# First-layer products of two feature tiles in 15 block products instead of 18, amid the last pair's second layer

## The chip, the cores and the metric

The kernel runs on one core of one Trainium2 chip. The metric is the device time of one launch in microseconds. TensorE (PE in the profile) does the matrix products, VectorE (DVE), ScalarE (ACT) and GpSimd (POOL) the elementwise work, and SyncE (SP) starts the transfers. The five run their own instruction lists and meet only at semaphores. An engine never passes over an instruction that waits: all that stands behind it in the list waits too.

## The reference

The program has three stages: an attention-like recurrence, four experts of two layers each with relu between them, and one wide block of two layers with a gate between them.

```python
def _moe_ref(x, domain_probs, w1, w2) -> np.ndarray:
    N, D = x.shape
    E = w1.shape[0]
    p = domain_probs / (domain_probs.sum(-1, keepdims=True) + 1e-09)
    out = np.zeros((N, D), dtype=np.float32)
    for e in range(E):
        h = np.maximum(x @ w1[e], 0.0)
        out += p[:, e:e + 1] * (h @ w2[e])
    return out.astype(np.float32)

def _moe2_ref(x, w_in, w_out) -> np.ndarray:
    h = x @ w_in
    g = h * (1.0 / (1.0 + np.exp(-1.702 * h)))
    return (g @ w_out).astype(np.float32)
```

There are N = 1536 tokens, D = 384 channels, E = 4 experts of F = 1024 features, and 2048 features in the last block. The change touches neither the recurrence nor expert 0.

## The kernel before

Everything is kept transposed: channels or features on the 128 partitions, tokens along the free axis. The 384 channels are 3 tiles (`KT`), the tokens 3 blocks of 512 (`NB`; expert 0 has the first of them in two spans of 256), and the features of an expert 8 tiles (`FT`). The last block counts as two more stages of 8 tiles. Single precision is made of two float32r parts, `hi` and `lo = x - hi`. A product of two such numbers is three matmuls: hi with hi, hi with lo, and lo with hi (`PASSES`, line 1068).

One step j is one feature tile on one block of tokens. `hidden(j)` (line 1078) is its first layer: 3 channel tiles x 3 passes = 9 matmuls of 512 columns into one of two banks of PSUM (`HID`). `output(j)` (line 1102) is its second layer, 9 matmuls into three banks that add up over all features of the block. PE's list goes hidden(j), output(j-1), hidden(j+1), ... Between the two stand ACT, which writes the relu's high part (line 700), and DVE, which writes its low part from PSUM (line 876). In the last block it is a sigmoid (706), a product (884), a copy (708) and a subtraction (886). After the features of a block DVE multiplies the output by the token's share `p_bc` into one of two `part` buffers (line 866), and POOL adds that to `acc` (631). POOL and ACT also split the next stage's weights into their parts, in pieces of 384 columns (622, 670), and after the last expert the new x (635, 717). The order of all this is written out in the code by loops over j, and for the recurrence by a table that the change leaves alone.

## Time and profile before

| | |
|---|---|
| time, median of 3 runs | 642.78 us (642.29 to 642.92) |
| profiled execution, its span | 640.5 us |
| PE busy | 635.2 us (99%) |
| DVE, ACT, POOL busy | 222.4, 203.4, 170.0 us (35, 32, 27%) |
| granted TensorE clock | 1.000 |

The span is that of one profiled execution, from its first instruction to its last; the time of a launch holds a little more. Busy shares are means over the whole span. An idle engine costs nothing unless another one waits for it. A matmul's listed length runs from its start to its modelled end, and the next one starts before that.

### The profile page before, as it was taken

How to read it: one execution, taken by the hardware profiler on the slowest of the kernel's cores; microseconds unless marked ns; L12 is line 12 of the kernel's file. 1: busy time of each engine (PE TensorE's matmuls, PEld its weight loads, DVE VectorE, ACT ScalarE, POOL GpSimd, SP SyncE). 2: the span in 40 equal slices, each digit the busy share in tenths (PEclk: the TensorE clock that was granted, in tenths of full speed). 3: DMA queues.
4: the chain of work that ended last, by engine and by line, in shares of the span. 5: the costliest groups of instructions: out<-in, count | busy, mean ns of one | idle time of the engine just before them, and what ended most of it. 6: DMA issues, size and time to landing. Idle time of an engine off the chain costs nothing.

```text
span 640.5 us, 9440 instructions
## 1 busy us (share of the span) xinstructions
PE 635.2 (99%) x3880; PEld 529.3 (83%) x3880; DVE 222.4 (35%) x369; ACT 203.4 (32%) x421; POOL 170.0 (27%) x168
## 2 busy tenths in 40 slices
PE   8999999999999999999999999999999999999998
PEld 6999888888888888888888888888888888888886
DVE  8987642212121212121212121213533333333332
ACT  4744432332222212222211223223643333333223
POOL 5664300342242303242402245422750000000000
PEclk9999999999999999999999999999999999999999
DMA  8765521006000501000310000220000010001001
GB/s 331 278 217 189 202 115 51 4 1 247 1 0 1 196 2 49 2 0 1 151 47 1 0 1 0 98 101 1 2 0 1 3 47 1 0 2 50 1 0 50
DMA packets 8722, 39.08 MB, mean 61 GB/s; under 512 B 1504, under 2 KB 1632, under 8 KB 7392
## 3 DMA queue, kind: packets, MB, share of 16 engines
q1 hardware_dynamic: 8672, 38.40, 15.9%
q8 instruction: 33, 0.54, 0.3%
q14 instruction: 17, 0.14, 0.1%
HBM read 36.01 MB, written 2.38 MB: 60 GB/s over the span
## 4 chain that ended last, share of the span: by engine, by line
PE 98%; DVE 1%; DMA 0%; issue 0%; ACT 0%; DVEq 0%
PE bank L1097 46%; PE bank L1123 31%; PE bank L1139 15%; PE bank L1171 2%; PE bank L1215 1%; PE bank L1218 1%; PE bank L1205 1%; PE bank L1190 1%; PE bank L1208 0%; DMA wu_sb<-wu_rows 0%; DVE w_pow L800 0%; DVE q_k_mid L816 0%; PE bank L1223 0%; DVE q_tab_k L807 0%; DVE acc L951 0%
## 5 line engine op out<-in xcount | busy, mean ns | idle before, releaser
L1097 PE MATMUL bank<-x_hi,w_hi 128*128 128x512 f32 (+1 forms) x456 | 172.5, 378 | 0.0
L1097 PE MATMUL bank<-x_lo,w_hi 128*128 128x512 f32 (+1 forms) x456 | 172.4, 378 | 0.0
L1097 PE MATMUL bank<-x_hi,w_lo 128*128 128x512 f32 (+1 forms) x456 | 172.3, 378 | 0.0
L876 DVE SCALAR_TENSOR_TENSOR h_lo<-bank,h_hi 128x512 fp32r<-128x512 f32 (+1 forms) x104 | 67.5, 649 | 257.3 <-ACT h_hi L700 257.3
L700 ACT ACTIVATE h_hi<-bank 128x512 fp32r<-128x512 f32 (+1 forms) x104 | 58.7, 564 | 286.6 <-PE bank L1097 286.6
L622 POOL TENSOR_TENSOR w_lo<-staging,w_hi 128x384 fp32r<-128x384 f32 x80 | 82.2, 1039 | 173.4 <-ACT w_hi L670 173.4
L1123 PE MATMUL bank<-h_hi,w_hi 128*128 128x512 f32 (+1 forms) x312 | 117.7, 377 | 0.1
L1123 PE MATMUL bank<-h_hi,w_lo 128*128 128x512 f32 (+1 forms) x312 | 116.3, 373 | 0.0
L1123 PE MATMUL bank<-h_lo,w_hi 128*128 128x512 f32 (+1 forms) x312 | 116.3, 373 | 0.0
L1097 PEld LDWEIGHTS bank<-x_hi,w_hi 128*128 128x128 f32 x456 | 85.8, 188 | 15.9
L1097 PEld LDWEIGHTS bank<-x_hi,w_lo 128*128 128x128 f32 x456 | 85.8, 188 | 15.8
L1097 PEld LDWEIGHTS bank<-x_lo,w_hi 128*128 128x128 f32 x456 | 85.8, 188 | 15.8
L1123 PEld LDWEIGHTS bank<-h_hi,w_hi 128*128 128x128 f32 x312 | 58.7, 188 | 12.1 <-issue 0.5
L1123 PEld LDWEIGHTS bank<-h_hi,w_lo 128*128 128x128 f32 x312 | 58.7, 188 | 10.3
L1123 PEld LDWEIGHTS bank<-h_lo,w_hi 128*128 128x128 f32 x312 | 58.7, 188 | 10.2
L884 DVE TENSOR_TENSOR acc<-bank,acc 128x512 f32<-128x512 f32 x48 | 33.2, 691 | 90.2 <-ACT acc L706 90.2
L631 POOL TENSOR_TENSOR acc<-acc,part 128x512 f32<-128x512 f32 x27 | 34.2, 1294 | 84.9 <-DVE part L866 84.9
L1139 PE MATMUL bank<-h_lo,w_hi 128*128 128x512 f32 x144 | 56.0, 389 | 0.0
L1139 PE MATMUL bank<-h_hi,w_hi 128*128 128x512 f32 x144 | 56.0, 389 | 0.0
L1139 PE MATMUL bank<-h_hi,w_lo 128*128 128x512 f32 x144 | 56.0, 389 | 0.0
L706 ACT ACTIVATE acc<-bank 128x512 f32<-128x512 f32 x48 | 28.7, 597 | 84.0 <-PE bank L1097 84.0
L670 ACT ACTIVATE w_hi<-staging 128x384 fp32r<-128x384 f32 x96 | 47.2, 516 | 2.9 <-DMA staging<-weights 2.9
(86 smaller groups left out, 433.4 us busy)
## 6 DMA issues: line engine op xcount, KB each, us to landing
staging<-weights SPq DMA_DIRECT2D x10, 1536.0 KB, 8.7
rkv_in<-rkv_n SPq DMA_DIRECT2D x10, 640.0 KB, 5.5
rk_in<-rk_t SPq DMA_DIRECT2D x12, 512.0 KB, 5.2
staging<-weights SPq DMA_DIRECT2D x4, 768.0 KB, 8.9
p_bc<-p_normalised SPq DMA_DIRECT2D x4, 768.0 KB, 4.2
out<-p_bc SPq DMA_DIRECT2D x9, 256.0 KB, 2.1
rkv_in<-rkv_n SPq DMA_DIRECT2D x2, 448.0 KB, 5.7
u_bc<-u_rows SPq DMA_DIRECT2D x1, 192.0 KB, 11.7
```

What stands on the lines that cost most here:

```text
L622: pool.tensor_tensor(part_of(w_lo[s % 2], f, piece), part_of(staging, f, piece), part_of(w_hi[s % 2], f, piece).bitcast(F32), ALU.subtract ...
L631: pool.tensor_tensor(acc[:, k, cols], acc[:, k, cols], part[:, i % 2, :], ALU.add).then_inc(sem["acc"], 1)
L670: act.activation(part_of(w_hi[s % 2], f, piece), part_of(staging, f, piece), ACT.Copy).then_inc(sem["whi"], 1)
L700: act.activation(h_hi[:, j % HRING, 0:size], hid, ACT.Relu).then_inc(sem["hhi"], 1)
L706: act.activation(sig[g % 2], hid, ACT.Sigmoid, scale=1.702).then_inc(sem["sig"], 1)
L876: dve.scalar_tensor_tensor(h_lo[:, slot, 0:size], hid, 0.0, h_hi[:, slot, 0:size].bitcast(F32), ALU.max, ALU.subtract).then_inc(sem["hlo"], 1)
L884: dve.tensor_tensor(gated[g % 2], hid, sig[g % 2], ALU.mult).then_inc(sem["gate"], 1)
L1097: last = pe.matmul(bank[:, HID[j % 2], 0:tokens.stop - tokens.start], w[:, k, :], xs[c][:, k, tokens], start=(n == 0), stop=(n == 3 * KT - 1))
L1123: last = pe.matmul(out_tile(n, k), w[:, k * P:(k + 1) * P], hs[c][:, slot, 0:size],   start=(first and i == 0 and not (n < SMALLS and k == ...
L1139: last = pe.matmul(out_tile(MOE_BLOCKS + b, k), w[:, k * P:(k + 1) * P], hs[c][:, slot, :], start=(first and i == 0), stop=(last_f and i = ...
L1171: last = pe.matmul(bank[:, a_banks(c)[g], p * P:(p + 1) * P], k_mid[rows, c % 2, p, :], r_mid[rows, c % R_RING, p, :], start=True, stop=True)
L1190: last = pe.matmul(kv_of(c)[rows, p * SW + g * D:p * SW + (g + 1) * D], kn_in[:, x, keys], v_in[:, x, p, V_ALL[g]], start=True, stop=True)
```

## The change

The features of experts 1 to 3 and of the last block are taken in pairs of two tiles: 12 pairs for the experts (`MOE_PAIRS`), 8 for the last block, 20 in all. For a pair, the first layer is a product of a 2 x 3 by a 3 x 3 array of blocks (2 feature tiles, 3 channel tiles, 3 blocks of tokens). Done plainly it has 18 block products; the new code does 15, by a scheme of Hopcroft and Kerr, and pair 12 (`PLAIN`) stays plain.

- A block product is three matmuls (`product`, line 1778). Its weight block is one of the tiles or one of 12 sums of tiles that DVE forms for each pair, 128 x 128 each (`weight_sums`, lines 1358 to 1373). Its token block is one of the blocks of x or one of 8 sums, formed once for the experts (`blocks0`) and once for the last block (`blocks1`) by `form` (13 operations on DVE, lines 1316 to 1346), and split by ACT (`sum_high`) and POOL (`sums_low`, line 811).
- The 15 products go into three banks of PSUM (`LONG`, `SHORT`, `ONE`) and are chained there: a product adds to what the bank holds. After each, ACT copies the bank into a tile in SBUF (`t_of`, 6 copies, line 1009) or DVE adds it to one (`join`, 9 additions, lines 1386 and 1388). The next product of the bank waits for that.
- The six finished tiles are then split by ACT and DVE (line 1431, experts), or pass the sigmoid, the gate (line 1425) and a split by ACT and POOL (line 843, last block). All of these read SBUF.
- The second layer of a pair goes in nine groups of six matmuls (`group`, line 1819), three for each block of tokens. For the first block the banks 0 to 2 keep adding up over the pairs of a stage. For the others, banks 3 and 4 in turn are emptied after each group (`leave`, DVE): in the experts through `part`, with `gather` on POOL (line 837), in the last block into `acc2`.
- `pairs()` writes one list for all four engines. In it the products of the next pair stand between the groups of the pair before (`mix`), and the elementwise work some places behind what it reads.

```diff
-SPANS += [(b * NB, NB) for e in range(1, E) for b in range(BLOCKS)]
...
+MOE_PAIRS = (E - 1) * PAIRS_E
+ALL_PAIRS = (STAGES - 1) * PAIRS_E
+PLAIN = MOE_PAIRS
+PRODUCTS = 15
+SUMS = 12
+T_RING, H_RING = 8, 9
...
+ONE, LONG, SHORT = 7, 5, 6
+PRODUCT = (
+    (0, (1, 1), ONE, True, "copy", 1, 1),
...
+    (11, (1, 2), LONG, False, "add", 2, 1),
+)
...
+SUM_ORDER = (13, 8, 14, 3, 9, 1, 10, 4)
...
+        def pairs():
+
+            order = [("product", 0, i) for i in range(PRODUCTS)]
+            begin = {0: 0}
+
+            def mix(q, lead):
+                begin[q + 1] = len(order)
+                left = iter(range(PRODUCTS))
+                for n, takes in enumerate(lead):
+                    if n:
+                        order.append(("group", q, *divmod(n - 1, KT)))
+                    order.extend(("product", q + 1, next(left)) for _ in range(takes))
+
+            for q in range(PLAIN - 1):
+                mix(q, (2, 1, 1, 2, 2, 2, 2, 1, 1, 1))
+            q = PLAIN - 1
+            begin[PLAIN] = len(order)
+            order += [("group", q, n, k) for n in range(2) for k in range(KT)] + [("plain", PLAIN, i) for i in range(2)]
+            order += [("group", q, 2, k) for k in range(KT)] + [("plain", PLAIN, i) for i in range(2, 6)]
+            mix(PLAIN, (0, 0, 0, 0, 0, 2, 1, 2, 2, 8))
+            for q in range(PLAIN + 1, ALL_PAIRS - 1):
+                mix(q, (2, 1, 1, 2, 2, 2, 2, 1, 1, 1))
+            begin[ALL_PAIRS] = len(order)
+            order += [("group", ALL_PAIRS - 1, n, k) for n in range(BLOCKS) for k in range(KT)]
+
+            after = [[] for _ in range(len(order) + 8)]
+            for at, (what, q, *rest) in enumerate(order):
+                if what == "product" and rest[0] in (LAST_OF[o] for o in DONE):
+                    pos = DONE.index(PRODUCT[rest[0]][5])
+                elif what == "plain":
+                    pos = rest[0]
+                else:
+                    if what == "group" and q == PLAIN - 1:
+                        after[at + 2].append(("rest", q, *rest))
+                    continue
+                later = iter(range(at + 1, at + 5))
+                if q >= MOE_PAIRS:
+                    after[next(later)].append(("silu", q, pos))
+                    after[next(later)].append(("gate", q, pos))
+                after[next(later)].append(("high", q, pos))
+                after[next(later)].append(("low", q, pos))
+            for q in range(1, ALL_PAIRS):
+                at = begin[q - 1]
+                if q == PLAIN:
+                    after[at + 4].append(("weight", q, 0))
+                else:
+                    for i, way in enumerate((0, 1, 2)):
+                        after[at + i].append(("sum", q, way))
+                    for i, piece in zip((3, 4, 5, 6, 7), range(len(PIECES))):
+                        after[at + i].append(("weight", q, piece))
+            for q in range(ALL_PAIRS):
+                after[begin[q] + 9].append(("second", q))
+            out = []
+            for at in range(len(after)):
+                out += order[at:at + 1] + after[at]
+            return out
...
-            def split_low(s, f, piece):
-                n = 2 * FT * (s - 1) + 2 * f + piece
-                pool.wait_ge(sem["whi"], 2 * FT + n + 1)
-                pool.tensor_tensor(part_of(w_lo[s % 2], f, piece), part_of(staging, f, piece),
-                                   part_of(w_hi[s % 2], f, piece).bitcast(F32), ALU.subtract).then_inc(sem["wlo"], 1)
-
-            def gather(n):
-
-                e, cols = expert_of(n), slice(SPANS[n][0], sum(SPANS[n]))
-                for k in range(KT):
-                    i = n * KT + k
-                    pool.wait_ge(sem["ev1"], i + 1)
-                    pool.tensor_tensor(acc[:, k, cols], acc[:, k, cols], part[:, i % 2, :], ALU.add).then_inc(sem["acc"], 1)
...
+            def sums_low(turn, blocks):
+
+                for i, op in enumerate(SUM_ORDER):
+                    pool.wait_ge(sem["shi"], len(SUM_ORDER) * turn + i + 1)
+                    pool.tensor_tensor(sum_home(s_lo, x_lo, op), blocks[FORMED[op][0]], sum_home(s_hi, x_hi, op).bitcast(F32),
+                                       ALU.subtract).then_inc(sem["slo"], 1)
...
+            def gather(q, n, k):
+
+                i = LEAVES[q, n, k]
+                pool.wait_ge(sem["evac"], i + 1)
+                cols = slice(n * NB, (n + 1) * NB)
+                pool.tensor_tensor(acc[:, k, cols], acc[:, k, cols], part[:, i % 2, :], ALU.add).then_inc(sem["gath"], 1)
...
+            second_low(0)
+            for what, q, *rest in PAIR_LIST:
+                if what == "group" and (q, *rest) in LEAVES and q < MOE_PAIRS:
+                    gather(q, *rest)
+                elif what == "weight":
+                    weight_low(q, *rest)
+                elif what == "second" and q:
+                    second_low(q)
+                elif what == "low" and q >= MOE_PAIRS:
+                    tile_low(q, *rest)
+                elif what == "plain" and rest[0] == 5:
+                    sums_low(1, blocks1)
...
+            def join(q, i):
+
+                _, _, at, _, _, o, sign = PRODUCT[i]
+                t = t_of[t_number(q, o) % T_RING]
+                before = [x for x in ADDED if x < i and PRODUCT[x][5] == o]
+                dve.wait_ge(sem["prod"], PRODS[q] + i + 1)
+                if before:
+                    dve.wait_ge(sem["added"], JOINED[q] + ADDED.index(before[-1]) + 1)
+                else:
+                    dve.wait_ge(sem["copied"], TAKEN[q] + COPY_OF.index(o) + 1)
+                if sign > 0:
+                    dve.tensor_tensor(t, bank[:, at, :], t, ALU.add).then_inc(sem["added"], 1)
+                else:
+                    dve.scalar_tensor_tensor(t, bank[:, at, :], -1.0, t, ALU.mult, ALU.add).then_inc(sem["added"], 1)
...
+            def leave(q, n, k):
+
+                i = LEAVES[q, n, k]
+                cols = slice(n * NB, (n + 1) * NB)
+                dve.wait_ge(sem["grp"], groups(q, n, k))
+                src = bank[:, KEPT[k] if n == 0 else shared_bank(q, n, k), :]
+                if q < MOE_PAIRS:
+                    if n == 1 and k == 0 or n == 0 and k == 0:
+                        dve.wait_ge(s_prob, 16 * (2 + q // PAIRS_E))
+                    if i >= 2:
+                        dve.wait_ge(sem["gath"], i - 1)
+                    dve.tensor_tensor(part[:, i % 2, :], src, p_bc[:, cols], ALU.mult).then_inc(sem["evac"], 1)
...
+                    dve.tensor_tensor(t, t, part[:, number % 2, :], ALU.mult).then_inc(sem["gate"], 1)
...
+                dve.scalar_tensor_tensor(tile_lo[number % H_RING], t_of[t_number(q, result_of(q, pos)) % T_RING], 0.0,
+                                         tile_hi[number % H_RING].bitcast(F32), ALU.max, ALU.subtract).then_inc(sem["tlo"], 1)
...
+                elif what == "plain" and rest[0] == 5:
+                    form(1, blocks1, 0, FORMINGS)
...
+            def product(q, i):
+
+                weight, rows, at, begins, _, _, _ = PRODUCT[i]
+                piece = next(n for n, (first, last) in enumerate(PIECES) if first <= weight < last)
+                pe.wait_ge(sem["alo"], PARTS_W[q] + piece + 1)
+                if q in (0, PLAIN + 1) and type(rows) is int:
+                    pe.wait_ge(sem["slo"], len(SUM_ORDER) * (q > 0) + SUM_ORDER.index(rows) + 1)
+                if q == PLAIN + 1 and begins and i < 3:
+                    pe.wait_ge(sem["gate"], 6)
+                earlier = [x for x in range(i) if PRODUCT[x][2] == at]
+                if earlier:
+                    x, before = earlier[-1], q
+                elif q and q != PLAIN + 1:
+                    x, before = max(x for x in range(PRODUCTS) if PRODUCT[x][2] == at), q - 1
+                else:
+                    x = None
+                if x in COPIED:
+                    pe.wait_ge(sem["copied"], TAKEN[before] + COPIED.index(x) + 1)
+                elif x in ADDED:
+                    pe.wait_ge(sem["added"], JOINED[before] + ADDED.index(x) + 1)
+                for n, (a, c) in enumerate(PASSES):
+                    last = pe.matmul(bank[:, at, :], a_parts[a][:, q % 2, weight * P:(weight + 1) * P], rows_of(ss[c], xs[c], rows),
+                                     start=(begins and n == 0), stop=(n == 2), skip_group_check=True)
+                last.then_inc(sem["prod"], 1)
...
+            def group(q, n, k):
+
+                begins, ends = (kept_first(q), kept_last(q)) if n == 0 else (True, True)
+                if n == 0:
+                    at = KEPT[k]
+                    if q == 0:
+                        pe.wait_ge(sem["ev1"], KT * len(SPANS))
+                    elif begins:
+                        pe.wait_ge(sem["evac"], LEAVES[q - 1, 0, k] + 1)
+                else:
+                    at = shared_bank(q, n, k)
+                    number = shared_number(q, n, k)
+                    if number >= len(SHARED):
+                        pe.wait_ge(sem["evac"], LEAVES[shared_at(number - len(SHARED))] + 1)
+                pe.wait_ge(sem["vlo"], q + 1)
+                for f in range(2):
+                    number = 6 * q + place_of(q, f, n)
+                    done, value = low_tile(number)
+                    pe.wait_ge(sem[done], value)
+                    for i, (a, c) in enumerate(PASSES):
+                        last = pe.matmul(bank[:, at, :], v_parts[a][q % 2][:, f * DM + k * P:f * DM + (k + 1) * P], tiles[c][number % H_RING],
+                                         start=(begins and f == 0 and i == 0), stop=(ends and f == 1 and i == 2))
+                last.then_inc(sem["grp"], 1)
+
```

How the order changes is shown at three places, by engine. `waits` names the semaphores.

PE. Before, nine matmuls of each layer alternate (`h_` is the hidden tile, `w_` the weights); the rows are the last three of an output and the first three of the next hidden tile.

```order
L1123 MATMUL bank<-h_hi,w_hi11 128x512
L1123 MATMUL bank<-h_lo,w_hi11 128x512
L1123 MATMUL bank<-h_hi,w_lo11 128x512
L1097 MATMUL bank<-x_hi,w_hi00 128x512 [waits s_hlo,s_wlo]
L1097 MATMUL bank<-x_lo,w_hi00 128x512
L1097 MATMUL bank<-x_hi,w_lo00 128x512
```

Now, the end of a pair's products and the start of the next: the last group of the pair before, product 14, and products 0 and 1 of the next pair (the `a_` tensors are the first layer's weights; the group reads hidden tiles and `w_hi00`, the second layer's weights). `s_added` is counted by DVE's joins, `s_tlo` by the tiles' low parts, `s_evac` by the leaves.

```order
L1819 MATMUL bank<-w_lo00,w_hi00 128x512 [waits s_tlo,s_vlo,s_evac]
L1819 MATMUL bank<-w_lo00,w_hi00 128x512 x2
L1819 MATMUL bank<-w_lo00,w_hi00 128x512 [waits s_tlo]
L1819 MATMUL bank<-w_lo00,w_hi00 128x512 x2
L1778 MATMUL bank<-x_hi,a_hi 128x512 [waits s_added,s_alo]
L1778 MATMUL bank<-x_lo,a_hi 128x512
L1778 MATMUL bank<-x_hi,a_lo 128x512
L1778 MATMUL bank<-x_hi,a_hi 128x512 [waits s_added,s_alo]
L1778 MATMUL bank<-x_lo,a_hi 128x512
L1778 MATMUL bank<-x_hi,a_lo 128x512
L1778 MATMUL bank<-s_hi,a_hi 128x512 [waits s_added,s_alo]
```

Each product now waits for the join or copy of the product before it on the same bank (the last row, product 1, for that of product 14, which stands one product back), and the groups wait for the tiles' low parts.

DVE, at the same place: joins (1386, 1388), leaves (1401), low parts of tiles (1431), and then the first of the 12 weight sums (1358 and on). Before, DVE had here only eight low parts in a row and three leaves.

```order
L876 SCALAR_TENSOR_TENSOR h_lo<-bank,h_hi 128x512 [waits s_hhi,s_l1] x8
L866 TENSOR_TENSOR part<-bank,p_bc0 128x512 [waits s_acc,s_prob0,s_l2]
L866 TENSOR_TENSOR part<-bank,p_bc0 128x512 [waits s_acc] x2
L876 SCALAR_TENSOR_TENSOR h_lo<-bank,h_hi 128x512 [waits s_hhi,s_l1] x8
L866 TENSOR_TENSOR part<-bank,p_bc1 128x512 [waits s_acc,s_prob1,s_l2]
```

```order
L1401 TENSOR_TENSOR part<-bank,p_bc 128x512 [waits s_gath,s_grp]
L1388 SCALAR_TENSOR_TENSOR t_rest<-bank,t_rest 128x512 [waits s_copied,s_prod]
L1431 SCALAR_TENSOR_TENSOR w_lo00<-t_most,w_lo00 128x512 [waits s_thi]
L1401 TENSOR_TENSOR part<-bank,p_bc 128x512 [waits s_gath,s_grp]
L1386 TENSOR_TENSOR t_most<-bank,t_most 128x512 [waits s_copied,s_prod]
L1431 SCALAR_TENSOR_TENSOR w_lo00<-t_rest,w_lo00 128x512 [waits s_thi]
L1358 TENSOR_TENSOR staging1<-staging0 128x128 [waits s_alo,s_first1]
L1359 TENSOR_TENSOR staging1<-staging0 128x128
L1361 TENSOR_TENSOR staging1<-staging1,staging0 128x128 [waits s_asum]
```

The join of product 14 (the last 1386) stands behind a leave and a low part, and each operation on a tile in SBUF stands between operations on PSUM.

POOL, at the switch from the experts to the last block. Before, the gathers (631), the new x (635), and the weights of the second half:

```order
L631 TENSOR_TENSOR acc<-acc,part 128x512 [waits s_ev1] x3
L635 TENSOR_TENSOR x_lo<-acc,x_hi 128x512 [waits s_xhi] x3
L631 TENSOR_TENSOR acc<-acc,part 128x512 [waits s_ev1] x3
L635 TENSOR_TENSOR x_lo<-acc,x_hi 128x512 [waits s_xhi] x3
L622 TENSOR_TENSOR w_lo10<-staging0,w_hi10 128x3x128 [waits s_whi]
```

Now: the last gather, the low parts of the plain pair's first two tiles (843), the low parts of the eight sums (811), and the low parts of its other four tiles.

```order
L837 TENSOR_TENSOR acc<-acc,part 128x512 [waits s_evac]
L843 TENSOR_TENSOR w_lo00<-t_most,w_lo00 128x512 [waits s_thi] x2
L811 TENSOR_TENSOR s_lo<-acc,s_hi 128x512 [waits s_shi] x6
L811 TENSOR_TENSOR x_lo<-acc,x_hi 128x512 [waits s_shi] x2
L843 TENSOR_TENSOR w_lo00<-t_most,w_lo00 128x512 [waits s_thi]
L843 TENSOR_TENSOR w_hi01<-t_most,w_hi01 128x512 [waits s_thi] x3
```

The eight low parts of the sums stand between the second and the third tile of the plain pair.

## Rows read from the trace of the kernel before

**Rows 1.** The page, part 1: busy time, share, instructions of each engine.

```profile
PE 635.2 (99%) x3880; PEld 529.3 (83%) x3880; DVE 222.4 (35%) x369; ACT 203.4 (32%) x421; POOL 170.0 (27%) x168
```

**Rows 2.** The page, part 4: shares of the chain that ended last.

```profile
PE 98%; DVE 1%; DMA 0%; issue 0%; ACT 0%; DVEq 0%
```

**Rows 3.** Whom PE waited for: us in total, times, longest.

```profile
PE bank L1053 <- POOL part L513: 1.4, 1, 1.4
PE bank L1171 <- DVE q_r_mid L819: 0.5, 2, 0.3
```

**Rows 4.** The chain in order of time: start, length (us), what.

```profile
502.72 2.04 PE bank L1097 x9
```

**Rows 5.** Groups by form, PE: count, busy us, mean ns, idle before.

```profile
L1097 PE MATMUL bank<-x_lo,w_hi 128*128 128x512 f32 x408 | 158.8, 389 | 0.0
L1139 PE MATMUL bank<-h_lo,w_hi 128*128 128x512 f32 x144 | 56.0, 389 | 0.0
```

**Rows 6.** Timeline of DVE, then POOL, 454 to 463 us: start, length, what.

```profile
455.41 1.43 DVE L886 TENSOR_TENSOR h_lo<-acc,h_hi 128x512 fp32r<-128x512 f32 x1 [0.70 <-ACT h_hi L708]
456.78 0.69 DVE L884 TENSOR_TENSOR acc<-bank,acc 128x512 f32<-128x512 f32 x1
458.17 1.06 DVE L886 TENSOR_TENSOR h_lo<-acc,h_hi 128x512 fp32r<-128x512 f32 x1 [0.70 <-ACT h_hi L708]
...
462.00 1.57 DVE L886 TENSOR_TENSOR h_lo<-acc,h_hi 128x512 fp32r<-128x512 f32 x1 [0.70 <-ACT h_hi L708]
...
454.98 1.31 POOL L635 TENSOR_TENSOR x_lo<-acc,x_hi 128x512 fp32r<-128x512 f32 x1
456.23 2.45 POOL L622 TENSOR_TENSOR w_lo<-staging,w_hi 128x384 fp32r<-128x384 f32 x2
```

**Rows 7.** Lines 884 and 886: ns min/median/max, first and last start.

```profile
L884 DVE TENSOR_TENSOR acc<-bank,acc x48: 681/692/693, 442.3 to 632.0; 128x512 f32<-128x512 f32 x48
...
L886 DVE TENSOR_TENSOR h_lo<-acc,h_hi x48: 691/693/1575, 443.6 to 633.4; 128x512 fp32r<-128x512 f32 x48
```

**Rows 8.** Timeline of POOL, 440 to 475 us: twelve splits without a gap.

```profile
456.23 13.55 POOL L622 TENSOR_TENSOR w_lo<-staging,w_hi 128x384 fp32r<-128x384 f32 x12
```

**Rows 9.** Lines 631 and 622 on POOL: ns min/median/max.

```profile
L631 POOL TENSOR_TENSOR acc<-acc,part x27: 1277/1295/1299, 183.2 to 447.5; 128x512 f32<-128x512 f32 x27
...
L622 POOL TENSOR_TENSOR w_lo<-staging,w_hi x80: 1002/1014/1475, 116.2 to 475.8; 128x384 fp32r<-128x384 f32 x80
```

**Rows 10.** Groups by form, DVE and ACT.

```profile
L876 DVE SCALAR_TENSOR_TENSOR h_lo<-bank,h_hi 128x512 fp32r<-128x512 f32 x88 | 60.8, 691 | 252.9 <-ACT h_hi L700 252.9
...
L708 ACT ACTIVATE h_hi<-acc 128x512 fp32r<-128x512 f32 x48 | 30.4, 633 | 40.1 <-DVE acc L884 40.1
L706 ACT ACTIVATE acc<-bank 128x512 f32<-128x512 f32 x48 | 28.7, 597 | 84.0 <-PE bank L1097 84.0
...
L866 DVE TENSOR_TENSOR part<-bank,p_bc 128x512 f32<-128x512 f32 x27 | 17.8, 687 | 12.5 <-POOL acc L631 7.3 <-PE bank L1123 5.2
...
L901 DVE TENSOR_TENSOR acc<-rkv_in,bank 128x128 f32<-128x128 f32 x1 | 0.3, 273 | 0.0
```

**Rows 11.** Timeline, 215 to 222.5 us: the end of an expert's block.

```profile
214.69 0.39 PE L1123 MATMUL bank<-h_hi,w_lo 128*128 128x512 f32 x1
...
215.12 1.29 DVE L866 TENSOR_TENSOR part<-bank,p_bc 128x512 f32<-128x512 f32 x2 [0.65 <-PE bank L1123]
...
215.89 3.79 POOL L631 TENSOR_TENSOR acc<-acc,part 128x512 f32<-128x512 f32 x3 [0.71 <-DVE part L866]
```

**Rows 12.** Line 932: ns min/median/max with one and with two inputs in SBUF.

```profile
L932 DVE SCALAR_TENSOR_TENSOR part<-part,w_pow,bank x20: 303/306/315, 21.4 to 68.0; 128x96 f32<-128x96 f32 x20
L932 DVE SCALAR_TENSOR_TENSOR part<-part,w_pow,late_kv x12: 310/314/319, 72.9 to 95.5; 128x96 f32<-128x96 f32 x12
```

**Rows 13.** Timeline of PE, 0 to 10 us: the first matmuls.

```profile
1.39 3.60 PE L1053 MATMUL bank<-part 128*128 128x512 bf16 x8 [1.39 <-POOL part L513]
```

**Rows 14.** The page, part 6: count, KB each, us to landing.

```profile
staging<-weights SPq DMA_DIRECT2D x10, 1536.0 KB, 8.7
...
p_bc<-p_normalised SPq DMA_DIRECT2D x4, 768.0 KB, 4.2
```

662 lines of the change are left out of this document (456 added, 206 removed).

## The prediction

> **What bounds the kernel now.** I read the busy shares first [rows 1], then the chain that ended last [rows 2], then who TensorE (PE) waited for [rows 3]. PE is busy for 99% of the span and carries 98% of the chain, and in 640.5 us it waits twice, 1.9 us together. VectorE (DVE) is at 35%, ScalarE (ACT) at 32%, GpSimd (POOL) at 27%. Nothing but PE's own stream sets the end. The reader should see one trap: a 512-column matmul is listed with 389 ns [rows 5], but nine of them take 2.04 us on the chain [rows 4]. They overlap, and each one costs 0.227 us. The median of the runs, 642.78 us, is 2.3 us above the span; I sum against the span and add 2.3.
>
> **What is removed.** P0 to P14 are the products of a pair of feature tiles, g0 to g8 its nine groups of six second-layer matmuls, q the pair's number. A product is 3 matmuls (0.68 us), a group 1.36 us. A pair had 54 first-layer matmuls and has 45; 19 of the 20 pairs change (pair 12 stays plain). 19 x 9 = 171 matmuls x 0.227 = **-38.8 us**. A pair falls from 108 x 0.227 = 24.5 to 22.4 us.
>
> **What is added, and the port.** Per pair DVE now has 9 joins, 6 leaves and 6 tile rests or gates, each 0.69 us [rows 10] with 0.60 from start to start when they stand in a row (two take 1.29 [rows 11]), and 12 sums of 128 columns at 0.27 [rows 10], 0.19 in a row with the same overlap: 21 x 0.60 + 12 x 0.19 = 14.9 us. POOL has six 512-column subtractions or gathers at 1.29 (1.28 in a row), three of 768 columns, and three of 128. From 384 columns at 1.014 and 512 at 1.295 [rows 9] those are 1.84 and 0.46: 7.7 + 5.5 + 1.4 = 14.6 us. ACT has up to 18 tile operations of 0.60 to 0.63 and six weight parts: under 15. All fit in 22.4 us, so no engine is the bound by its sum.
> One thing changes that [rows 6 to 8]. A DVE operation with both inputs in SBUF (L886) has a median of 0.693 us, but 1.43, 1.06 and 1.57 where POOL is running. At 455.41 it lasts until POOL's operation of 454.98 has ended (456.29), plus 0.6. L884, with one input in PSUM, is 0.69 at 456.78 beside the same POOL work, and never above 0.693 in 48 [rows 7]. POOL in turn takes 2.45 us for two operations of 1.01 [rows 6], and 1.13 each over twelve [rows 8]. So such DVE operations and POOL's run one at a time, and the waiting one comes next. The new tile rests, gates, weight sums and block sums are all of this kind, while the rests before (L876) read PSUM. The Trainium skill, page "SBUF — State Buffer", section "Who interferes with whom", says just this: a VectorE instruction with two SBUF inputs contends with a GpSimd one that reads SBUF, and one with at most one SBUF input does not. It speaks against this change; by its opposite the sum is rival A's.
> A second rule would cost more: the "Vector Engine (DVE) Microarchitecture Reference", section "Points that are easy to get wrong", holds that a scalar_tensor_tensor with two non-bf16 SBUF sources runs at half throughput. By it each of the 72 new tile rests of the expert pairs would take about 0.5 us more, and the 11 expert seams, as an estimate, up to 5.5 us together, 673 in the sum. The row disagrees: L932 takes 310 to 319 ns with two SBUF inputs and 303 to 315 with one [rows 12]. I leave it out.
>
> **Seams between pairs.** P1 of the next pair needs the bank of P14, and only P0 (0.68 us) stands between. A consumer starts 0.43 us after the start of the last matmul [rows 11], 0.20 after it would give way to the next; join 14 then takes 0.69. With DVE free P1 starts 0.25 us late. With the port, from the end of P14 as 0: the rest of P11's tile waits for gather g6 until -2.55 and ends -1.95; leave g7 ends -1.27; gather g7 holds the port from -1.23 to 0.05; the rest of P12's tile runs to 0.65, leave g8 to 1.25, join 14 to 1.85. P1 starts 1.2 us late. Bounds 0.25 and 1.2; 11 expert seams, taken at 1.1: **+12.1**. In the last stage POOL's tile rest sits in the gather's place and leaves 0.5: 6 x 0.5 = **+3.0**. After P14 there is room (g0 to g8), so other banks are free in time.
> At the two expert ends (pairs 3 and 7) three more gathers stand before the weight splits. Gathers are then up to 1.5 us late where a leave needs one of two `part` buffers, and the next seam inherits it: 0.5 to 3 each, taken at 1.5: **+3.0**. P7 to P14 of pair 13 stand in a row: **+1.0** (0.5 to 1.5).
>
> **Before pair 0.** In the last block of expert 0, DVE's last four block sums alternate with POOL's first s_lo rests (1.28 us each), so the hidden rest of step 28 ends 2.5 us after PE wants it; 0 to 2.5, taken **+1.5**. Pair 0's products have no groups between. DVE's 12 sums for pair 1 stand before join 3 and wait until pair 0's weights are split, 2.7 us after P0 starts. POOL goes straight on with 1.84 us of second weights, so the sums end at 6.9, join 3 at 7.6, and P6 starts then instead of 3.6. With 0.6 more in the chain: **+4.5** (2.5 if the port were free).
>
> **The switch to the last stage.** Time 0 is the end of P14 of pair 11. PE's own work up to the end of the plain pair is 24.5 us, and to g3 of pair 12 it is 28.6. Plain tiles 0 and 1 need the first block of x: leave (DVE), gather (POOL, 1.28), high part (ACT, 0.63), rest (DVE, two SBUF inputs). DVE has pair 13's 12 weight sums between these, all on the port. By the queues in their order: leave g0 ends 3.8, gather 5.2; leave g1 6.5, gather 7.8; leave g2 9.7, gather 11.0; leave g3 13.3, gather 14.6; the rests of the first block end 11.6, 15.2 and 16.3. Plain 0 starts at 16.4, not 8.2. POOL's first 768-column split waits for ACT, which has the high part of g3 before it (15.2); gathers g4 and g5 end 20.0 and 23.0, g6 (behind the other splits) 28.3, g8 (behind the second-layer split) 34.7. The last rest ends 36.6, and plain 4 and 5 end 40.8: 16.3 late.
> Then DVE's 13 block sums run from 37.9 to 46.0, before the gates of tiles 3 to 5 (48.8). ACT's high part of tile 5 ends 49.4, the first sum's 50.0. POOL's list has the eight s_lo rests before the rests of plain tiles 2 and 3: 8 x 1.28 + 1.6 for the port = 61.9, and two more to 64.5. PE has done g0 to g2 and needs both for g3. So g3 is 64.5 - 28.6 = **+36** late. With a free port the same queues give 32.9 and 54.1: 25.5. I take the port's value, since L886 is stretched in all the rows that meet POOL.
> **Clock.** The kernel's first eight 512-column matmuls take 3.60 us, 0.45 each, though the granted clock reads 1.00 [rows 13]: twice 0.227. PE will now stand idle for 8, 7 and 20 us. If it comes back as at the start, each costs some 1.8: 0 to 5.4, taken **+3.0**.
> Loads are no term: weights land 8.7 us after issue for 1536 KB [rows 14], a pair takes 384 KB twice, over a period ahead. The shares `p_bc` lose their second buffer, but a load lands in 4.2 us and g3 is 10 us off. The tail swaps a 0.60 us copy for a 0.69 us addition.
>
> **Sum.** -38.8 + 12.1 + 3.0 + 3.0 + 1.0 + 1.5 + 4.5 + 36 + 3.0 = +25.3. 640.5 + 25.3 + 2.3 = **668 us**.
>
> **Rivals.**
> A, on the other side: the port doesn't bind, because small or scalar_tensor_tensor operations slip in, or POOL's gaps meet them. Then seams 17 x 0.25 = 4.3, expert ends 1.0, pair 13 0.5, pair 0 2.5, switch 25.5, clock 2: 35.8, so -3.0, 640 us. It decides as soon as all stalls stay under 38.8 us, which needs the switch below some 30. For it: no row shows a scalar_tensor_tensor meeting POOL. Against: [rows 6, 7].
> B: DVE becomes the bound. With 14.9 us of work and 18 port operations a pair, each waiting a full 0.9 us, an expert pair takes 31 us; even 2 us more than I have, over 11 pairs, gives 690. For: DVE serves everything in list order. Against: seam to seam I find POOL idle for some 8 us.
> C: the port is free and the second half of the switch is hidden as well: A's 640 less the 17.1 between 8.4 and 25.5 = 623. Against: PE's list has g3 next, with nothing to pass it.
> That fewer matmuls run than said, or more, I give nothing: the list has 45 for each of the 19 pairs.
>
> **From these to the numbers.** Forecast 0.65, own range 652 to 684; A 0.20; B 0.07; C 0.08. A measurement of this kernel can tell 0.2% (1.3 us) from no change. A splits into 0.15 faster, 0.04 same and 0.01 slower; C is faster; the forecast and B are slower. Faster 0.23, same 0.04, slower 0.73. The range 634 to 686 leaves out C and most of B.
>
> **What would show it.** PE has 3709 matmuls and waits of some 50 to 60 us in all: one of about 20 us before L1819 on POOL's L843, near 490 us, one of about 8 before L1795 on DVE's L1438 and one of about 7 before the fifth plain tile. Seams show as waits of 0.5 to 1.3 us before L1778 on DVE's joins (L1386, L1388), 17 times. L1431 and L1425 have a median near 0.7 and a maximum above 1.8. If L1431 never passes 0.7, the port is wrong and A holds. If PE's wait at L1819 is under 10 us, the list at the switch was misread; if seams are above 2 us, B.

## The result: 5.6% slower, as forecast, by 10 us more than forecast

The changed kernel takes 678.14 us (median of 4 runs, 676.78 to 679.32), the kernel before 642.53 (642.24 to 642.92): ratio 1.0555, 95% interval 1.0539 to 1.0571. Forecast were 668.0 us, 634 to 686, and slower at 0.73. In the profiled execution the span went from 640.5 to 674.9 us, +34.4.

The page of the changed kernel, part 1 (beside [rows 1]) and the shares of the chain (beside [rows 2]):

```profile
span 674.9 us, 10722 instructions
PE 617.0 (91%) x3709; PEld 500.4 (74%) x3709; DVE 502.8 (75%) x864; ACT 294.2 (44%) x578; POOL 388.3 (58%) x318
PE 61%; DVE 18%; POOL 10%; issue 8%; ACT 3%; DMA 1%; DVEq 0%; ACTq 0%; SPq 0%
```

There are 171 matmuls fewer, as planned. But VectorE now has 864 instructions and not 369, and TensorE, which carried 98% of the chain, carries 61%. For whom TensorE waited (us in total, times, longest), beside [rows 3]:

```profile
PE bank L1778 <- DVE t_most L1386: 15.1, 18, 2.8
PE bank L1819 <- POOL w_lo L843: 13.0, 1, 13.0
PE bank L1819 <- DVE part L1401: 6.2, 2, 5.6
PE bank L1795 <- DVE x_lo L1438: 6.1, 1, 6.1
PE bank L1778 <- DVE t_rest L1386: 4.7, 6, 1.1
PE bank L1778 <- DVE t_most L1388: 3.4, 4, 2.7
PE bank L1549 <- DVE h_lo L1148: 1.6, 1, 1.6
```

These seven rows hold 50.1 us; before, it was 1.9 in two. The waits before L1778 are banks that a join has not left yet, 28 of them. The 1.6 stands in the last block of expert 0, ahead of the pairs; the others are the switch to the last stage.

The port, which [rows 6, 7] showed for one form only, is there for the others with two inputs in SBUF. Lines 1431 (rests of the experts' tiles), 1425 (gates) and 1372 (a weight sum), minimum, median and maximum in ns, with L1386 (one input in PSUM) last:

```profile
L1431 DVE SCALAR_TENSOR_TENSOR w_lo<-t_most,w_lo x36: 680/1378/1745, 158.9 to 436.8; 128x512 fp32r<-128x512 f32 x36
L1425 DVE TENSOR_TENSOR t_most<-t_most,part x30: 678/1130/1914, 507.3 to 663.1; 128x512 f32<-128x512 f32 x30
L1372 DVE TENSOR_TENSOR staging<-staging x19: 279/284/1932, 144.6 to 618.1; 128x128 f32<-128x128 f32 x19
L1386 DVE TENSOR_TENSOR t_most<-bank,t_most x70: 674/689/692, 157.5 to 659.7; 128x512 f32<-128x512 f32 x70
```

For L1431 the median is twice the minimum, for L1425 1.7 times: 45 of all 72 rests and 21 of all 42 gates took over 1 us. I had expected medians near 0.7, and a maximum above 1.8, which L1425 has and L1431 (1.745) has not. The weight sums meet GpSimd seldom: 14 of 228 took over 1 us, nearly all the others 0.28.

An expert seam, the end of an expert, and a pair of the last stage in TensorE's timeline (start, length, and in brackets the wait before it), the rows with a wait alone:

```profile
189.65 0.47 PE L1778 MATMUL bank<-s_hi,a_hi 128*128 128x512 f32 x1 [1.08 <-DVE t_most L1386]
213.47 0.47 PE L1778 MATMUL bank<-s_hi,a_hi 128*128 128x512 f32 x1 [1.09 <-DVE t_rest L1386]
...
237.27 0.47 PE L1778 MATMUL bank<-s_hi,a_hi 128*128 128x512 f32 x1 [1.07 <-DVE t_most L1386]
262.74 0.47 PE L1778 MATMUL bank<-s_hi,a_hi 128*128 128x512 f32 x1 [2.78 <-DVE t_most L1386]
...
359.51 0.47 PE L1778 MATMUL bank<-s_hi,a_hi 128*128 128x512 f32 x1 [2.78 <-DVE t_most L1386]
384.87 0.47 PE L1778 MATMUL bank<-s_hi,a_hi 128*128 128x512 f32 x1 [1.08 <-DVE t_most L1386]
...
563.07 0.47 PE L1778 MATMUL bank<-s_hi,a_hi 128*128 128x512 f32 x1 [0.56 <-DVE t_most L1386]
572.39 0.47 PE L1778 MATMUL bank<-s_hi,a_hi 128*128 128x512 f32 x1 [0.23 <-DVE t_most L1388]
575.81 0.47 PE L1778 MATMUL bank<-s_hi,a_hi 128*128 128x512 f32 x1 [0.32 <-DVE t_most L1386]
587.53 0.47 PE L1778 MATMUL bank<-s_hi,a_hi 128*128 128x512 f32 x1 [0.56 <-DVE t_most L1386]
```

A pair is 99 matmuls, 22.44 us at 0.2267. From P1 to P1 it takes 23.82 in an expert, 25.47 over an expert's end (237.27 to 262.74) and 24.46 in the last stage, which has three gaps and not one. A gap costs some 0.25 us more than its length: it counts from a modelled end, 0.39 us after the start of a matmul whose successor would have come at 0.227, and the first matmul after it is followed 0.31 later. I call this 0.25 the restart.

The switch. First TensorE's waits there, then what ran on VectorE, ScalarE and GpSimd in its second half:

```profile
443.06 1.65 PE L1819 MATMUL bank<-w_hi 128*128 128x512 f32 x3 [5.61 <-DVE part L1401]
454.73 1.66 PE L1819 MATMUL bank<-w_lo,w_hi 128*128 128x512 f32 x6 [0.58 <-DVE part L1401]
466.61 0.77 PE L1795 MATMUL bank<-x_hi,a_hi 128*128 128x512 f32 x1 [6.14 <-DVE x_lo L1438]
...
474.85 0.69 DVE L1346 TENSOR_TENSOR acc<-acc 128x512 f32<-128x512 f32 x1
475.46 1.28 DVE L1423 TENSOR_TENSOR t_most<-bank,t_most 128x512 f32<-128x512 f32 x2
478.78 3.21 ACT L973 ACTIVATE s_hi<-acc 128x512 fp32r<-128x512 f32 x6
479.47 7.54 POOL L811 TENSOR_TENSOR s_lo<-acc,s_hi 128x512 fp32r<-128x512 f32 x6 [11.83 <-ACT s_hi L973]
486.96 2.48 POOL L811 TENSOR_TENSOR x_lo<-acc,x_hi 128x512 fp32r<-128x512 f32 x2
489.40 1.26 POOL L843 TENSOR_TENSOR w_lo<-t_most,w_lo 128x512 fp32r<-128x512 f32 x1
490.62 1.27 POOL L843 TENSOR_TENSOR w_hi<-t_most,w_hi 128x512 fp32r<-128x512 f32 x1
490.81 0.77 PE L1819 MATMUL bank<-w_lo,w_hi 128*128 128x512 f32 x1 [12.97 <-POOL w_lo L843]
```

It is the queue that the forecast walked through: block sums, gates, high parts, eight rests, and only then the two rests for the fourth group. The clock behind the waits, in the windows' columns (us, busy PE, PEld, DVE, ACT, POOL, granted clock, DMA share, GB/s):

```profile
443.00:446.00 3.00, 2.94 (x7) 2.39 (x8) 2.28 (x4) 1.24 (x2) 1.65 (x1) 0.50 0.00 0
449.00:464.00 15.00, 10.89 (x47) 8.35 (x45) 5.76 (x9) 7.48 (x13) 10.85 (x10) 1.00 0.08 26
467.00:470.00 3.00, 3.00 (x8) 2.35 (x8) 3.00 (x6) 0.63 (x1) 0.64 (x1) 0.50 0.00 0
491.00:494.00 3.00, 3.00 (x8) 2.27 (x9) 0.25 (x1) 0.00 (x0) 3.00 (x3) 0.50 0.03 5
```

After each of the three long waits the granted clock reads 0.50, that is 1.2 GHz, and the next 13 or 14 matmuls start 0.43 us apart, not 0.227. That costs 2.74, 2.89 and 2.73 us, 8.4 in all.

### The profile page after: what moved, and what is told of

It reads as the page before. It is cut to its first block, busy times and chain, and to the rows that moved or that the text cites. A ratio compares the mean times of both kernels' runs of the same rounds, so it can differ in the third digit from the quotient of the medians.

```text
span 674.9 us, 10722 instructions
## 1 busy us (share of the span) xinstructions
PE 617.0 (91%) x3709; PEld 500.4 (74%) x3709; DVE 502.8 (75%) x864; ACT 294.2 (44%) x578; POOL 388.3 (58%) x318
## 4 chain that ended last, share of the span: by engine, by line
PE 61%; DVE 18%; POOL 10%; issue 8%; ACT 3%; DMA 1%; DVEq 0%; ACTq 0%; SPq 0%
PE bank L1819 22%; PE bank L1778 18%; PE bank L1524 7%; PE bank L1549 7%; POOL acc L837 4%; POOL a_lo L825 3%; DVE t_most L1425 2%; DVE part L1401 2%; PE bank L1580 2%; DVE t_most L1386 2%; DVE w_lo L1431 2%; DVE t_most L1388 2%; DVE staging L1372 1%; POOL s_lo L811 1%; POOL w_hi L830 1%
## 5 line engine op out<-in xcount | busy, mean ns | idle before, releaser
L1819 PE MATMUL bank<-w_lo,w_hi 128*128 128x512 f32 x729 | 189.2, 393 | 13.6 <-POOL w_lo L843 13.0
L1819 PEld LDWEIGHTS bank<-w_lo,w_hi 128*128 128x128 f32 x729 | 137.8, 190 | 44.0 <-issue 13.4
L837 POOL TENSOR_TENSOR acc<-acc,part 128x512 f32<-128x512 f32 x81 | 116.0, 1435 | 62.1 <-DVE part L1401 62.1
L825 POOL TENSOR_TENSOR a_lo<-staging,a_hi 128x128 fp32r<-128x128 f32 (+1 forms) x96 | 100.9, 1081 | 58.9 <-ACT a_hi L990 55.1
L1819 PE MATMUL bank<-w_hi 128*128 128x512 f32 x351 | 95.2, 400 | 5.6 <-DVE part L1401 5.6
L1819 PEld LDWEIGHTS bank<-w_hi 128*128 128x128 f32 x351 | 67.9, 194 | 20.5 <-DVE part L1401 6.0
L1401 DVE TENSOR_TENSOR part<-bank,p_bc 128x512 f32<-128x512 f32 x81 | 55.6, 686 | 35.5 <-PE bank L1819 29.8
L1778 PE MATMUL bank<-s_hi,a_hi 128*128 128x512 f32 x114 | 47.2, 414 | 24.8 <-DVE t_most L1386 14.7
L1009 ACT ACTIVATE t_most<-bank 128x512 f32<-128x512 f32 x84 | 49.7, 593 | 42.5 <-PE bank L1778 41.5
L1778 PE MATMUL bank<-x_hi,a_hi 128*128 128x512 f32 x171 | 67.2, 393 | 0.5 <-DVE t_most L1386 0.4
L1778 PE MATMUL bank<-x_lo,a_hi 128*128 128x512 f32 x171 | 66.6, 390 | 0.0
L1778 PE MATMUL bank<-x_hi,a_lo 128*128 128x512 f32 x171 | 66.6, 389 | 0.0
L1388 DVE SCALAR_TENSOR_TENSOR t_most<-bank,t_most 128x512 f32<-128x512 f32 x56 | 38.5, 688 | 19.5 <-PE bank L1778 18.5
L1778 PEld LDWEIGHTS bank<-s_hi,a_hi 128*128 128x128 f32 x114 | 21.4, 187 | 41.6 <-issue 31.3
L1386 DVE TENSOR_TENSOR t_most<-bank,t_most 128x512 f32<-128x512 f32 x70 | 48.0, 686 | 1.4 <-ACT t_most L1009 1.3
L990 ACT ACTIVATE a_hi<-staging 128x128 fp32r<-128x128 f32 (+1 forms) x95 | 42.5, 514 | 12.7 <-DVE staging L1373 9.7
L1778 PE MATMUL bank<-s_hi,a_lo 128*128 128x512 f32 x114 | 44.8, 393 | 0.0
L1778 PE MATMUL bank<-s_lo,a_hi 128*128 128x512 f32 x114 | 44.7, 392 | 0.0
L1431 DVE SCALAR_TENSOR_TENSOR w_lo<-t_most,w_lo 128x512 fp32r<-128x512 f32 x36 | 41.6, 1155 | 0.7 <-ACT w_lo L1038 0.6
```

Source lines behind the costliest of these rows:

```text
L825: pool.tensor_tensor(new, src, high.bitcast(F32), ALU.subtract).then_inc(sem["alo"], 1)
L837: pool.tensor_tensor(acc[:, k, cols], acc[:, k, cols], part[:, i % 2, :], ALU.add).then_inc(sem["gath"], 1)
L990: act.activation(a_hi[:, q % 2, first * P:last * P], src, ACT.Copy).then_inc(sem["ahi"], 1)
L1009: act.activation(t_of[number % T_RING], bank[:, at, :], ACT.Copy, scale=float(sign)).then_inc(sem["copied"], 1)
L1386: dve.tensor_tensor(t, bank[:, at, :], t, ALU.add).then_inc(sem["added"], 1)
L1388: dve.scalar_tensor_tensor(t, bank[:, at, :], -1.0, t, ALU.mult, ALU.add).then_inc(sem["added"], 1)
```

## The experiments

P0 to P14 are the fifteen block products of a pair. All times stand against the kernel before, run on the same chip (642.33 to 642.64 in each comparison).

**A group between P0 and P1.**

```diff
-                mix(q, (2, 1, 1, 2, 2, 2, 2, 1, 1, 1))
+                mix(q, (1, 2, 1, 2, 2, 2, 2, 1, 1, 1))
```

and the same in the last stage's loop.

> Edit: in each pair's mixed stretch a second-layer group stands between the first two block products (P0, group, P1) instead of P0, P1, group, so that 1.36 us of other matmuls stand ahead of the product whose bank the join of the last pair's P13 frees. Theory T1 (the wait is the distance between a bank's two uses, with a DVE that has room): the 11 expert seams of 1.08 us and the three gaps at expert ends and the pair-0 hand-off's first shrink to under 0.3 each, and the last stage's first gap of 0.56 goes; 11 x 1.3 + 2 x 2.4 + 6 x 0.8 = about -20 us, so 655 to 662 us, ratio to the kernel before about 1.025. Rival R1 (the joins come late because VectorE's accesses of about 1.3 us each behind GpSimd set the pace of the whole pair): the wait only moves to the next product, the seam stays at 0.8 to 1.1 in some other place, time 674 to 678.

663.51 us (662.76 to 664.37), ratio 1.0335 (1.0317 to 1.0352): 14.6 us back. The seams inside an expert are gone, at an expert's end 1.70 us are left, and the last stage has new waits:

```profile
352.18 0.47 PE L1778 MATMUL bank<-s_hi,a_hi 128*128 128x512 f32 x1 [1.70 <-DVE t_most L1386]
...
559.24 0.47 PE L1778 MATMUL bank<-s_hi,a_hi 128*128 128x512 f32 x1 [0.99 <-DVE t_most L1388]
562.64 0.47 PE L1778 MATMUL bank<-s_hi,a_hi 128*128 128x512 f32 x1 [0.31 <-DVE t_most L1386]
```

So the seam is a matter of distance between two uses of a bank, as T1 said. The bank is the one that the join of P14 frees; the expectation names P13 by mistake. T1 asked for too much beside it: the gaps at the expert ends (1.68 and 1.70 left) and at pair 0 (2.75) do not fall under 0.3, and the time is above its range. In the last stage R1 holds in part: a pair still loses 1.3 us plus two restarts, now before P6 and P8.

**The low parts before the block rests.** On GpSimd's list:

```diff
                 elif what == "low" and q >= MOE_PAIRS:
                     tile_low(q, *rest)
-                elif what == "plain" and rest[0] == 5:
-                    sums_low(1, blocks1)
+                    if q == PLAIN and rest[0] == 5:
+                        sums_low(1, blocks1)
```

> Edit: at the switch to the last stage GpSimd takes the low parts of plain pair's six feature tiles (through L843) ahead of the six block rests (L811), not behind them. Theory T1 (the wait of 12.97 us before the fourth second-layer group is the queue of GpSimd: six rests of 1.27 us = 7.5 us and two long splits stand before the low part awaited): the wait before L1819 on L843 falls by 7 to 10 us, the rests of the block sums come later but have groups in front of them; part of it comes back as a wait before L1778 on L811. Time 665 to 671, -7 to -13. Rival R2 (the wait is set by the gates and block sums on VectorE, and the rests are needed next anyway): under 3 us gained, the 12.97 splits into two waits of the same sum.

669.93 us (669.66 to 671.04), ratio 1.0435 (1.0417 to 1.0452): 8.2 us back. The wait of 12.97 is 0.8, and 2.4 and 1.1 have come in its place:

```profile
PE bank L1778 <- issue: 2.4, 1, 2.4
...
PE bank L1819 <- DVE p_bc L1411: 1.1, 1, 1.1
PE bank L1819 <- POOL w_hi L843: 0.8, 1, 0.8
```

**GpSimd only writes.** Left out: the low parts are zeros and the experts are not summed.

```diff
-                pool.tensor_tensor(tile_lo[number % H_RING], t_of[t_number(q, result_of(q, pos)) % T_RING],
-                                   tile_hi[number % H_RING].bitcast(F32), ALU.subtract).then_inc(sem["tlop"], 1)
+                fill(tile_lo[number % H_RING], NB).then_inc(sem["tlop"], 1)
```

where `fill` is three memsets, one after the other, two of the whole tile and one of half of it; and the same in L811, L825, L830 and L837.

> Edit: from the sums of blocks on, GpSimd's subtractions and gathers (two inputs from SBUF) are each replaced by three memsets of the same tile, which only write; the low parts then hold zeros and the experts are not summed, so the output is left out. Everything else, waits and counts included, stands. Theory T1 (VectorE's operations with two SBUF inputs take 1.3 to 1.9 us and not 0.68 because GpSimd's two-input operations hold what both read through): L1431's median falls from 1.35 to 0.68 to 0.75, VectorE's busy time falls by some 60 us or more, the seams before L1778 fall from 1.08 to under 0.4, and the three gaps of each last-stage pair go: 645 to 658 us. Rival R3 (VectorE's time is its own, or GpSimd's writes hold it as much as its reads): L1431 keeps a median over 1.1 and the time stays at 670 to 678.

651.05 us (650.09 to 652.08), ratio 1.0132 (1.0115 to 1.0149): 27.1 us less. The page, part 1, and lines 1439 and 1446, which are L1431 and L1438 of before the edit:

```profile
PE 612.1 (94%) x3709; PEld 500.1 (77%) x3709; DVE 433.6 (67%) x864; ACT 293.4 (45%) x578; POOL 382.0 (59%) x840
...
L1439 DVE SCALAR_TENSOR_TENSOR w_lo<-t_most,w_lo x36: 677/683/693, 156.6 to 421.2; 128x512 fp32r<-128x512 f32 x36
...
L1446 DVE TENSOR_TENSOR x_lo<-acc,x_hi x9: 676/681/693, 423.0 to 448.1; 128x512 fp32r<-128x512 f32 x9
```

GpSimd is as busy as before (382.0 against 388.3), yet VectorE's same 864 instructions take 433.6 us, not 502.8, and none of the pairs' is stretched. It is GpSimd's reading that holds them. The Trainium skill, page "SBUF — State Buffer", section "Who interferes with whom", says that a two-input instruction contends with GpSimd's reads and not with its writes; by that rule the edit frees VectorE, and this trace agrees, maximum 695 ns over the 72 rests of the experts' tiles. Nor is a scalar_tensor_tensor (L1439) slower than a tensor_tensor (L1446) by itself, so the second rule that the forecast weighed was rightly left out.

The wait that grew most is the fourth group's, 15.4 us against 13.0. Counted from the start of the fifth plain tile, TensorE came to it 0.9 us sooner and GpSimd's queue, with three memsets for each subtraction, ended 1.5 later.

**Short gates in the last stage.** Left out: 448 of 512 columns of the gate's product there.

```diff
-                    dve.tensor_tensor(t, t, part[:, number % 2, :], ALU.mult)
+                    dve.tensor_tensor(t[:, 0:64], t[:, 0:64], part[:, number % 2, 0:64], ALU.mult)
```

> Edit: in the last stage (not in the plain pair) the gate's product takes 64 of its 512 columns; the rest of the gating is left out. VectorE so has 42 operations shorter by about 1 us each there, with order, waits and counts as they were. Theory T1 (the three gaps of 0.56, 0.22 and 0.32 us in each last-stage pair come from VectorE being 82% busy there, so joins come late): VectorE's share in 530 to 675 falls to under 70%, the second and third gap go and the first falls under 0.3; a pair takes 22.5 to 22.9 instead of 24.46, time 664 to 669. Rival R4 (the gaps come from bank distance alone, or from the chain join, silu, gate, high, low behind ScalarE): a pair keeps over 24 us, time within 3 us of 678.

672.12 us (672.0 to 672.72), ratio 1.0467 (1.045 to 1.0485): 6.0 us less, not 9 to 14. From the fourth group to the end it takes 177.0 us against 184.1 (670.1 - 493.1 and 674.9 - 490.8); 2.3 us were lost before it, 1.4 of them to the clock at 263.62 (last section). The median is above the range of T1 too. VectorE, in the windows 515 to 640 us, short gates first:

```profile
515.00:640.00 125.00, 122.91 (x535) 99.36 (x534) 97.22 (x173) 70.68 (x130) 78.54 (x64) 1.00 0.08 23
```

```profile
515.00:640.00 125.00, 119.57 (x510) 93.87 (x509) 108.18 (x167) 67.44 (x125) 81.94 (x63) 1.00 0.08 23
```

78% instead of 87%, where I had expected under 70; from pair 15 on the gaps before P6 and P8 are gone, the first falls from 0.56 to 0.20, and a pair takes 22.9 us:

```profile
586.50 0.47 PE L1778 MATMUL bank<-s_hi,a_hi 128*128 128x512 f32 x1 [0.20 <-DVE t_most L1386]
609.41 0.47 PE L1778 MATMUL bank<-s_hi,a_hi 128*128 128x512 f32 x1 [0.20 <-DVE t_most L1386]
```

So those gaps are VectorE's lateness; R4 falls.

**The first two edits together.**

> Edit: the first two edits together (a group between P0 and P1; at the switch GpSimd takes the plain pair's low parts before the block rests). Theory T1 (two separate causes at separate places): the gains add, 678.1 - 14.6 - 8.2 = 655.3, so 654 to 657 us. Rival: they overlap at the switch, since in the first of them the wait before L1819 on L843 rose to 14.5 us and that hides there what comes earlier; then under 3 us below the first edit alone, 660 to 663.

655.89 us (655.04 to 656.89), ratio 1.0207 (1.019 to 1.0224). They add, to 0.6 us.

**Pair 13's weight sums eight places later** (with the two):

```diff
+                    late = 8 if q == PLAIN + 1 else 0
                     for i, way in enumerate((0, 1, 2)):
-                        after[at + i].append(("sum", q, way))
+                        after[at + late + i].append(("sum", q, way))
                     for i, piece in zip((3, 4, 5, 6, 7), range(len(PIECES))):
-                        after[at + i].append(("weight", q, piece))
+                        after[at + late + i].append(("weight", q, piece))
```

> Edit: the former two, and pair 13's twelve weight sums and their splits stand eight places later in the list, behind the hand-over of the gathered blocks. Theory T1 (in the first half of the switch VectorE's evictions L1401 stand behind weight sums of 1.35 us each and GpSimd's gathers L837 behind the splits L825): the waits of 5.6 (L1819 on L1401) and 6.1 us (L1795 on L1438) fall by 2 to 4 us in all, and the slow clock that follows them by 1; part comes back behind the fifth plain tile; 650 to 654 us against 655 for the two edits. Rival R5 (the chain eviction, gather, high part, rest of about 3.3 us a block sets it, whatever else is queued): no change within 1 us of the two edits, or a loss of 2 to 5 us as the sums collide with the forming of the blocks in the second half.

656.08 us (653.44 to 658.3), ratio 1.0198 (1.0168 to 1.0227): nothing gained, as R5 had it. The wait of 5.6 fell to 1.9, as T1 said, and one of 8.5 stands before the fifth plain tile instead of 6.1.

**The fourth gate amid the block sums** (with the first two edits):

```diff
                 elif what == "gate":
                     tile_gate(q, *rest)
+                    if q == PLAIN and rest[0] == 3:
+                        form(1, blocks1, 6, FORMINGS)
...
-                    form(1, blocks1, 0, FORMINGS)
+                    form(1, blocks1, 0, 6)
```

> Edit: the first two, and VectorE takes the gate of the plain pair's fourth tile after six of the thirteen block sums, not after all. Theory T1 (with the low parts first, the fourth group still waits for the gates, which stand behind 4 to 9 us of block sums): the plain pair's fourth tile is ready 4 us sooner, some of it is given back since the last sums come as much later; 652 to 655 us. Rival R6 (the sums' rests are what ends last, before the seventh and eighth group): time as for the two edits or 1 us worse.

658.04 us (657.8 to 658.33), ratio 1.0243 (1.0226 to 1.026): 2 us worse than the two. T1 is refuted; R6 is nearer, though it had at most 1 us. The fourth group's wait fell from 1.05 to 0.56, and the sixth group waits 4.2 us, where it waited 1.1, for the bank that a copy of VectorE (L1411) leaves.

**All of these, and pair 12's second-layer split behind the last gather.**

> Edit: all the edits before it, and the second-layer weights' split of the plain pair two places later, behind the last gather. Theory T1: the gains of the two halves of the switch add to those of the first two edits, 647 to 651 us, still above the kernel before's 642.4, because the last stage's pairs and the forming of sums over again remain. Rival: a piece moved late in the first half collides with the second, 652 to 657 us. Both put it above the kernel before.

654.61 us (653.57 to 657.68), ratio 1.0195 (1.0162 to 1.0227): no gain that can be told from the first two edits. Its timeline shows why the first half gave it back:

```profile
443.70 0.63 ACT L1046 ACTIVATE x_hi<-acc 128x512 fp32r<-128x512 f32 x1 [1.73 <-POOL acc L838]
...
445.01 1.36 DVE L1372 TENSOR_TENSOR staging<-staging 128x128 f32<-128x128 f32 x1
...
448.11 1.88 DVE L1374 TENSOR_TENSOR staging<-staging 128x128 f32<-128x128 f32 x1
...
449.91 1.79 DVE L1439 TENSOR_TENSOR x_lo<-acc,x_hi 128x512 fp32r<-128x512 f32 x2
```

The high part of the block is there at 444.3; its rest starts at 449.9, behind weight sums of 128 columns that take 1.4 to 1.9 us each beside GpSimd, where alone they take 0.28.

**The sums behind that rest, and the block sums whole again.** `late` is 11 for the sums and 9 for their splits.

> Edit: lead and low parts as in the two edits together; the plain pair's second-layer split two places later; pair 13's weight sums on VectorE eleven places later (behind the last gathered block's rest), their splits nine later; the block sums in one piece again. Theory T1 (when the sums stood eight places later they lay right in front of the last two x_lo rests: one x_hi was there at 444.3 and its rest began at 449.9, behind five sums of 1.35 to 1.89 us, and PE waited 9 us before the fifth plain tile): that wait falls from 9 to 3 to 5 us, the first stays near 1.9 instead of 5.6; against the two edits alone (655.9) 648 to 652 us. Rival R7 (whatever is taken out of the first half of the switch must be done in the second, where VectorE has to form the block sums and gates): the fifth plain tile comes sooner but the fourth group waits as much longer, 654 to 657 us.

657.88 us (655.25 to 659.55), ratio 1.0246 (1.0224 to 1.0267). The median is 2.0 above the first two edits, and the ranges overlap. R7 holds in kind: the fifth plain tile waits 5.3 instead of 9.05, but 3.9 and 2.0 come before the fourth and a later group and 2.7 further on. Work moved out of one half of the switch is paid in the other.

**Another order in the last stage** (on top of that):

```diff
             for q in range(PLAIN + 1, ALL_PAIRS - 1):
-                mix(q, (1, 2, 1, 2, 2, 2, 2, 1, 1, 1))
+                mix(q, (1, 2, 1, 1, 1, 2, 2, 2, 2, 1))
```

> Edit: as the one before it, and in the last stage's pairs the block products stand as 1,2,1,1,1,2,2,2,2,1 among the nine groups instead of 1,2,1,2,2,2,2,1,1,1: two groups, not one, and P4 and P5 between them, separate P3 from P6, whose bank P3's join frees. Theory T1 (the gaps of 1.0 and 0.31 us before P6 and P8 come from where VectorE's queue stands at that point, not from its total load of some 80%): both gaps go, 6 x 1.3 = 8 us less than the kernel before it. Rival R8 (VectorE's load there sets the pace, whatever the order): the wait turns up before P11 or P12 or at the next seam, within 2 us of the kernel before it.

652.47 us (651.3 to 655.5), ratio 1.0165 (1.0135 to 1.0195), 5.4 below the one before it, not 8. The waits on L1388 went from 5.7 us to 2.7, those on L1386 from 6.1 to 4.6; waits of up to 0.4 us on ScalarE's copies (L1009) came in. A pair takes 23.60 us, not 24.46. So the queue's place in the list decided 0.9 of the 2.0 us that a pair lost, with VectorE about as loaded as before (82% against 85% from 505 to 640 us); R8 falls. Between P3 and P6 the new order has three groups and two products, not the two groups of the expectation; the order before it had two and two.

**The three edits that gained.** P0, group, P1; the low parts first; the last stage's order.

> Edit: the first two edits (a group between P0 and P1; the low parts before the block rests) and the last stage's order 1,2,1,1,1,2,2,2,2,1, with the weight sums of pair 13 where the changed kernel has them. Theory T1 (the gains of separate places add, and moving the weight sums gained nothing): 655.9 - 5.4 = 650.5 us, 649 to 652, still 1.0% over the kernel before. Rival: it ties with the kernel before within 0.3% (641 to 645), which would need 6 us more than the places just named held.

653.77 us (653.72 to 656.62), ratio 1.019 (1.0165 to 1.0214): above the 649 to 652 expected, and above the kernel before. By the medians the last stage's order gave only 2.1 us here. No correct variant beats the kernel before; the interval of the best, 1.0135 to 1.0195, is clear of 1.

**The same, with GpSimd only writing** (left out as above).

> Edit: the same, with GpSimd's subtractions and gathers replaced by memsets that only write, as once before (low parts are zeros and the experts are not summed, so the output is left out). Theory T1 (what is still lost against the kernel before is mostly VectorE slowed by GpSimd's reads): 651.0 for the writes alone, less 9 to 12 for the low parts first (its wait of 15.4 us was that one), less 1 to 2 for the two orders: 637 to 642 us, at or under the kernel before. Rival R9 (the chain of operations at the switch costs as much whatever they take): 645 to 650 us, at most 5 us under the same kernel with subtractions.

632.43 us (632.3 to 633.3), ratio 0.9847 (0.9831 to 0.9864). 21.3 us less than the same kernel with subtractions, and less than the kernel before; R9 falls, and T1 (637 to 642) asked for too little. From pair 15 to pair 18 TensorE then loses nothing. With a GpSimd that only writes this order would win by 1.5%; with its reads none of the nine correct orders did.

## Why the prediction was right, and where its size was off

By stage, in us over the pure matmul time (2.04 / 9 = 0.2267 us for each). The last column takes differences of TensorE's starts in the trace, less what the kernel before has up to the same place.

| step of the forecast | forecast | measured |
|---|---|---|
| 171 matmuls fewer | -38.8 | -38.8 |
| last block of expert 0, and pair 0 up to P1 of pair 1 (165.9) | 1.5 + 4.5 | 7.4 |
| expert pairs, P1 to P1: 165.87 to 408.64, ten of 22.44 | 12.1 + 3.0 | 18.4 |
| switch, up to the fourth group of pair 12 | 36 + 3 | 31.9 |
| last stage from there | 1.0 + 3.0 | 15.5 |
| sum | +25.3 | +34.4 |

The matmuls saved are shown by their number. The waits of the first measured term (1.58, 2.74, 0.22, 0.47, 0.20, 0.27) sum to 5.5; restarts and shorter stops are the rest.

*The port.* Right, and stronger than I took it. The forecast had an operation with two SBUF inputs meeting GpSimd now and then, with medians near 0.7; 45 of 72 tile rests and 21 of 42 gates took over 1 us. The kernel with memsets shows it: the same instructions, 69 us less of VectorE, 27 us less in all. Rival A needed a port that doesn't bind; with such a port this kernel gives 651.05, where A said 640, so even A's condition would not have made it faster with its lists as they were: its four waits at the switch still sum to 25.3 us.

*Expert pairs.* The mechanism (P1 waits for the bank that the join of P14 frees) is shown by the group put in between. The wait was right, 1.08 for 1.1; the restart of 0.25 us a gap was not in the sum. At an expert's end the extra over a seam was 1.65 for 1.5. One of the pairs after it lost 1.6 us to the clock.

*The switch.* The second and third wait came at the place and by the releaser forecast, and the hand-overs at nearly the time: g3 at 60.4 after the same zero (430.4), forecast 64.5; plain 0 at 15.4 for 16.4, the last rest at 36.1 for 36.6. The first wait was put before plain 0, on its rest; it stands one group ahead of it, on a leave (L1401), and plain 0 follows without a wait. The forecast's own queue had that leave at 13.3, measured 12.7, and no term for the group that needs it. The waits are 25.3 of the 31.9, the slow clock after the first two 5.6 and restarts the rest. So the waits were taken too long, some 26 us with restarts for 36. The clock was taken too cheap: 3.0, at most 5.4, for three waits, where it cost 8.4, of which 2.7 stand in the last stage's row. Eight slow matmuls after each wait were assumed, and it was 13 or 14. The wait of 12.97 was forecast as "about 20"; the low-parts edit shows that its cause was the order on GpSimd's list, though only 8.2 of it could be had.

*The step that failed in size* is "the last stage's seams, 6 x 0.5". The 15.5 of the last row are 2.7 of slow clock, 1.3 at pair 13 (forecast 1.0) and 11.5 in the six pairs, 8.5 more than forecast. Of the 11.5, 4.5 stand at the seams before P1, with restarts, and 7.0 further on in the pairs, for which the forecast had no term. The other errors nearly cancel, to +0.6 of the 9.1 by which the sum was short: +1.4 at the start, +3.3 at the expert pairs, +0.3 at pair 13, +5.4 for the clock, -9.8 for the waits at the switch. That the time came out within 1.5% of the forecast is partly luck. I had looked for one wait a pair, at the seam, and not asked what VectorE's queue does in the middle of the pair. VectorE has as many operations a pair there as in the experts, but is busy for 87% (515 to 640 us) and not 77% (290 to 382), and it is late at P6 and P8 as well. The short gates show that it is load, and the last order that a part of it is only position.

*The ends.* "VectorE becomes the bound" (B) needed seams above 2 us; none but the expert's end has that. C needed both a free port and a hidden second half; the kernel that comes nearest gives 632.43, where C said 623.

By the medians the last stage's order gave 5.4 us in one pair of kernels and 2.1 in another. Within that stage the traces show one number: from pair 15 on, the time over the pure matmuls falls from 9.21 to 5.49 us in the one and from 9.20 to 5.53 in the other. The rest of the difference lies ahead of it and within the 3 to 4 us by which one kernel's runs spread; what sets that spread stays open, and so does why VectorE is busier in the last stage than in the experts.

## What to carry to other kernels

Where a change takes 4% of the bound engine's work away and doubles another engine's, price each new operation at what it takes beside its neighbours, not at its minimum: TensorE's waits here, 54.3 us in all, fall to 34.7 when the operations of 0.68 us no longer take 1.3. Add what the clock costs after a long wait, here 2.7 to 2.9 us each time. Look for waits at every place where a buffer is used again within a pair and not at the seam alone, and put the wait's length in matmuls between the two uses. And when a transition is a serial chain through three engines, moving pieces within it gave between a gain of 1 us and a loss of 2 in four tries; taking a later need out of the queue's front gave 8.

## What the runs showed of the hardware

A VectorE operation with two SBUF inputs can lose as much to GpSimd's read when it is short: 128 columns took 0.28 us alone and up to 1.93 beside GpSimd. It happened to few, 14 of 228.

The clock after a wait of about 2.8 us isn't the same each time. In the changed kernel the wait before 262.74 was followed by a normal pair (23.76 us to the next P1), the equal one before 359.51 by a pair of 25.36, with the granted clock at 0.69 in the window after it:

```profile
359.50:365.00 5.50, 5.49 (x17) 4.43 (x18) 4.20 (x14) 2.08 (x4) 0.62 (x1) 0.69 0.34 143
```

With short gates the first one did it:

```profile
263.62 0.76 PE L1778 MATMUL bank<-s_hi,a_hi 128*128 128x512 f32 x1 [2.77 <-DVE t_most L1386]
288.78 0.47 PE L1778 MATMUL bank<-s_hi,a_hi 128*128 128x512 f32 x1 [1.08 <-DVE t_most L1386]
```

25.16 us, with a first matmul of 0.76, and the second one too (25.37 us after 361.80). With the low parts first both did, at 263.66 and 362.05 (25.40 and 25.39 us). The seams' waits of 1.08 never did it. That each such wait may or may not cost 1.5 us might explain why some kernels with waits spread over 4 to 5 us and the kernel before over 0.9. But one with them (the fourth gate amid the sums) spread over 0.5 only, and the mean granted clock of the runs does not settle it: with later sums the fastest run has 0.987 (653.44 us) and one of the slow ones 0.981 (657.49), but with the three edits 0.979 and 0.984 go with 653.76 and 653.78. So that link is argued and not shown.
